# Expert routing on one core: the key's 32 bits searched in six digits in place of seven

## The reference, cut to what matters

```
logits = x @ w_gate                       # 2304 x 8
order  = argsort(-logits.flatten())
cap    = 2304 // 8                        # 288 tokens for each expert
for idx in order:                         # highest logit first
    tok, e = idx // 8, idx % 8
    if tok is assigned or expert e is full: continue
    assign tok to e
out[tokens of e] = relu(x[tokens of e] @ w1[e]) @ w2[e]
```

## Time and profile before

| what | value |
|---|---|
| median of 3 runs | 928.96 us (927.03 to 929.26) |
| the profiled execution | 927.07 us |
| its span, first to last instruction | 925.4 us |
| PE busy | 834.3 us, 90% of the span |
| DVE busy | 608.5 us, 66% |
| ACT busy | 351.6 us, 38% |
| POOL busy | 315.0 us, 34% |
| mean granted TensorE clock | 0.933 of full speed |

### The profile page before, as it was taken

One profiled execution on the slowest core, in us unless ns is written; L12 is line 12 of the kernel. 1 busy time (PEld: TensorE's weight loads), 2 busy tenths in 40 slices (PEclk: granted clock), 3 DMA queues, 4 the chain that ended last, 5 costly groups with the idle time before them and its releaser, 6 DMA issues. The chain is left out here.

```text
span 925.4 us, 21404 instructions
## 1 busy us (share of the span) xinstructions
PE 834.3 (90%) x7720; PEld 757.0 (82%) x7720; DVE 608.5 (66%) x1613; ACT 351.6 (38%) x856; POOL 315.0 (34%) x325
## 2 busy tenths in 40 slices
PE   4776999999999999999999999825999999999984
PEld 3656888888889888888898999724989999999984
DVE  5886886777778767876555555466766766766520
ACT  3453333443344333433323232203445355355451
POOL 5442220221122202211000000006676786786781
PEclk9756999998999999999999999955999999999998
DMA  7873132132221320311101000005614614615600
GB/s 184 257 203 116 40 90 75 27 80 81 62 76 38 88 75 20 80 51 36 46 2 45 0 23 1 24 2 206 206 64 174 228 64 174 229 64 172 230 29 26
DMA packets 97183, 85.40 MB, mean 92 GB/s; under 512 B 64625, under 2 KB 68721, under 8 KB 97137
## 3 DMA queue, kind: packets, MB, share of 16 engines
q1 hardware_dynamic: 94064, 75.34, 26.6%
q0 software_dynamic: 3072, 9.44, 3.2%
HBM read 70.60 MB, written 14.16 MB: 92 GB/s over the span
## 5 line engine op out<-in xcount | busy, mean ns | idle before, releaser
L451 PE MATMUL PS<-xs,W 128*128 128x256 f32 x1728 | 235.6, 289 | 0.2 <-issue 0.2
L451 PEld LDWEIGHTS PS<-xs,W 128*128 128x128 f32 x1728 | 225.2, 195 | 12.0 <-issue 3.9
L451 PE MATMUL PS<-W,g 128*128 128x512 f32 x864 | 223.1, 397 | 0.0
L451 PEld LDWEIGHTS PS<-W,g 128*128 128x128 f32 x864 | 153.7, 188 | 28.3 <-issue 1.0
L541 ACT ACTIVATE a_sb<-PS,one 128x256 f32<-128x256 f32 x144 | 68.2, 474 | 252.1 <-PE PS L451 252.1
L564 DVE TENSOR_SCALAR scratch<-a_sb 128x256 f32<-128x256 f32 x144 | 52.6, 365 | 95.1 <-ACT a_sb L541 95.1
L372 POOL TENSOR_TENSOR P<-P,top 128x640 f32<-128x640 f32 x16 | 21.1, 1316 | 254.3 <-DVE top L332 254.3
L1252 POOL TENSOR_TENSOR w1s<-w1r,w1s 128x512 fp32r<-128x512 f32 x64 | 80.4, 1284 | 29.3 <-ACT w1s L1163 29.1
L1092 PE MATMUL PS<-exs,w1s 128*128 128x288 f32 x256 | 83.1, 325 | 4.9 <-DVE ehs L1217 4.9
L1268 POOL TENSOR_TENSOR w2s<-w2r,w2s 128x512 fp32r<-128x512 f32 x64 | 80.9, 1283 | 17.6 <-ACT w2s L1187 17.4
L1092 PE MATMUL PS<-ehs,w2s 128*128 128x288 f32 x256 | 80.7, 315 | 1.1 <-POOL w2s L1268 1.1
(11 more groups left out here) (166 smaller groups left out, 1426.0 us busy)
## 6 DMA issues: line engine op xcount, KB each, us to landing
w1r<-in_moe_w SPq DMA_DIRECT2D x16, 1024.0 KB, 6.0
w2r<-in_moe_w SPq DMA_DIRECT2D x8, 2048.0 KB, 9.2
qn<-in_q SPq DMA_DIRECT2D x32, 144.0 KB, 3.8
kn<-in_k SPq DMA_DIRECT2D x32, 144.0 KB, 3.6
vd<-in_v SPq DMA_DIRECT2D x16, 288.0 KB
xt<-xT SPq DMA_DIRECT2D x16, 288.0 KB, 2.2
y<-scratch SPq DMA_DIRECT2D x18, 256.0 KB, 2.0
vw<-in_v SPq DMA_DIRECT2D x68, 64.0 KB, 2.4
```

Of the source, the lines that this page charges most:

```text
L451: r = pe.matmul(psum, wsel(w[i]), xsel(x[j]), start=first and t == 0, stop=last and t == 2)
```

## The change

The digits have 5, 5, 5, 5, 6 and 6 bits. Digits 4 and 5 have 64 thresholds each, so their `dve_over` has 18 x 64 = 1152 elements. There is one digit less for each assignment. The digits of steps 3 to 20 are placed anew: digit 3 stays at 3 and 5, digit 4 moves from 9 and 10 to 10 and 12, digit 5 from 14 and 15 to 18 and 19, and digit 6, which had 19 and 20, is gone. With it `dve_choose` moves from step 20 to 19 and `dve_ahead` from 23 to 22. POOL now clears all of `over`, 1216 elements, in place of its tail of 96. `unit` has 768 elements in place of 896, and the table of thresholds 6 x 64 in place of 7 x 32.

```
-DIG = 7
-RADIX = 32
+BITS = (5, 5, 5, 5, 6, 6)
+DIG = len(BITS)
+RADIX = [1 << b for b in BITS]
+MOST = max(RADIX)
+SHIFT = [32 - sum(BITS[:i + 1]) for i in range(DIG)]
+UNIT = [2.0 ** -sum(BITS[1:i + 1]) for i in range(DIG)]
...
-                for t, pattern, base, step in ((con["thr"], [[0, DIG], [1, RADIX]], 1, 0), (con["rev"], [[-1, E]], E, 0),
+                for t, pattern, base, step in ((con["thr"], [[0, DIG], [1, MOST]], 1, 0), (con["rev"], [[-1, E]], E, 0),
...
-        over = sb("over", [128, TILES * RADIX + 128 - RADIX], BF16)
-        over_t = over[:, 0:TILES * RADIX].rearrange("p (t k) -> p t k", t=TILES)
+        over = sb("over", [128, max((TILES - 1) * k + 128 for k in RADIX)], BF16)
+        over_t = [over[:, 0:TILES * k].rearrange("p (t k) -> p t k", t=TILES) for k in RADIX]
...
         def dve_over(dve, i):
-            dve.tensor_tensor(over_t, wide(rest_p, RADIX),
-                              thr[:, i, :].unsqueeze(1).to_broadcast([128, TILES, RADIX]), ALU.is_ge).then_inc(over_ready, 1)
+            k = RADIX[i]
+            dve.tensor_tensor(over_t[i], wide(rest_p, k),
+                              thr[:, i, 0:k].unsqueeze(1).to_broadcast([128, TILES, k]), ALU.is_ge).then_inc(over_ready, 1)
...
-                t = dve.tensor_scalar(digi[:, i, :], key_p, max(27 - 5 * i, 0), RADIX - 1 if i < DIG - 1 else 3,
+                t = dve.tensor_scalar(digi[:, i, :], key_p, SHIFT[i], RADIX[i] - 1,
...
-            dve.tensor_scalar(full[0:RADIX, :], cnt[0:RADIX, 0:E], float(CAP), None, ALU.is_ge).then_inc(full_ready, 1)
+            dve.tensor_scalar(full[0:RADIX[i], :], cnt[0:RADIX[i], 0:E], float(CAP), None, ALU.is_ge).then_inc(full_ready, 1)
...
-                x = pe.matmul(cnt[:, 0:E], over[:, t * RADIX:t * RADIX + 128], hot[:, t, :], start=t == 0, stop=t == TILES - 1)
+                x = pe.matmul(cnt[:, 0:E], over[:, t * RADIX[i]:t * RADIX[i] + 128], hot[:, t, :], start=t == 0, stop=t == TILES - 1)
...
-        COUNT = [49, 55, 60, 3, 9, 14, 19]
-        SUM = [51, 57, 62, 5, 10, 15, 20]
+        COUNT = [49, 55, 60, 3, 10, 18]
+        SUM = [51, 57, 62, 5, 12, 19]
...
-                for t in (unit[:, :, :], full[:, :], rows[:, 2:3], over[:, TILES * RADIX:], oneh[:, TILES * GP:]):
+                for t in (unit[:, :, :], full[:, :], rows[:, 2:3], over[:, :], oneh[:, TILES * GP:]):
...
-KEY_CHAIN, CHAIN = 5, 36
+KEY_CHAIN, CHAIN = 5, 34
```

More of the change, by code:

```diff
@@ L69, in network @@
         con = {}
-        for name, shape, dt in (("thr", [128, DIG, RADIX], F32),
+        for name, shape, dt in (("thr", [128, DIG, MOST], F32),
                                 ("rev", [128, E], F32),
@@ L718, in _ @@
                 for i in range(DIG):
-                    t = pool.memset(con["weight"][:, i, :], float(RADIX) ** -i)
+                    t = pool.memset(con["weight"][:, i, :], UNIT[i])
                 t.then_inc(con_ready, 1)
@@ L793, in _ @@
                 for i in range(1, DIG):
-                    t = dve.tensor_scalar(con["thr"][:, i, :], con["thr"][:, i, :], 1.0 if i == DIG - 1 else 0.0, float(RADIX) ** -i,
+                    t = dve.tensor_scalar(con["thr"][:, i, :], con["thr"][:, i, :], 1.0 if i == DIG - 1 else 0.0, UNIT[i],
                                           ALU.subtract, ALU.mult)
@@ L964, in dve_hot @@
             link(dve, m, dve.tensor_tensor(eq[:, :, :], eq[:, :, :], revb, ALU.mult))
-            dve.tensor_scalar(digi[:, 0, :], key_p, 27, None, ALU.arith_shift_right)
+            dve.tensor_scalar(digi[:, 0, :], key_p, SHIFT[0], None, ALU.arith_shift_right)
             link(dve, m, dve.tensor_reduce(pick[:, :], eq[:, :, :], AX.X, ALU.max))
-            dve.tensor_scalar(rest_p, digi[:, 0, :], 16.0, None, ALU.add)
+            dve.tensor_scalar(rest_p, digi[:, 0, :], RADIX[0] / 2.0, None, ALU.add)
             link(dve, m, dve.tensor_tensor(pick[:, :], pick[:, :], alive_p, ALU.mult))
@@ L995, in dve_choose @@
         def dve_choose(dve, m):
-            dve.tensor_scalar(rest_p, rest_p, kstar[:, 0:1], float(RADIX) ** -(DIG - 1), ALU.subtract, ALU.add)
+            dve.tensor_scalar(rest_p, rest_p, kstar[:, 0:1], UNIT[DIG - 1], ALU.subtract, ALU.add)
             link(dve, m, dve.scalar_tensor_tensor(fe[:, :], tot[:, 0:E], kstar[:, 0:1], con["rev"][:, :], ALU.is_equal, ALU.mult))
@@ L1304, in _ @@
                 for i in range(DIG):
-                    pool.memset(unit[0:RADIX, i, :], float(RADIX) ** -i).then_inc(init, 1)
+                    pool.memset(unit[0:RADIX[i], i, :], UNIT[i]).then_inc(init, 1)
                 pool.affine_select(out=below[:, :], in_=ones[:, :], compare_op=ALU.is_gt, fill=0.0, base=0,
```

## The result

| | before | after |
|---|---|---|
| median | 929.05 us (927.03 to 935.22, 6 runs) | 958.1 us (955.58 to 962.08, 6 runs) |
| the profiled execution | 927.07 us | 956.23 us |
| its span | 925.4 us | 954.5 us |
| clearing by POOL to the end | 325.0 us | 352.2 us |
| mean granted TensorE clock | 0.933 | 0.924 |

The ratio is 1.0305, 95% interval 1.0274 to 1.0336. The prediction was 924.2 us, "faster" with a chance of 0.75. It was wrong in sign, and the time lies far outside its range of 921.8 to 928.9.

A forecast was written before the change was run, and what follows sets the result against it. PE's queue was taken to set the rounds, with step 28 waiting for DVE's ehs(5). Terms -4.5 + 0.3 - 0.55 + 0.05 = -4.7 took 927.07 to 922.4; the median's 1.9 gave 924.2 us, range 921.8 to 928.9.

The forecast's parts named there:

- Is POOL's lock open earlier?: Rounds 1 to 6: `mem`, starting 0.50 ahead of POOL's fourth `w2s` end, gets in there, ending 1.25 us earlier.
- the prediction had 0.87: PE's stall in front of step 28, waiting for DVE's ehs(5): stays at 0.87, with step 28 0.75 us earlier.
- being tied to the steps ahead of 3: POOL's `w2s` borders in a round: set by steps ahead of 3, which were taken as unmoved.
- Rival 1: POOL's lock isn't open at the first border; `mem` ends with the fifth `w2s`; six rounds cost +3.0, 931.8 us; chance 0.13.
- A digit costs PE 0.68: PE's queue, rounds 0 to 6: count 0.55 plus sum 0.13 leave, 4.8 us in all if PE had no other limit.
- `mem` starts earlier: Round 3, step 3 to `mem`: 0.20 from ehs(4) and 0.20 from `kstar` going first, 0.40 us earlier.
- The wide comparison: DVE's 1152-element comparisons: 1.36 us each, 0.60 more, just fitting ahead of their counts; cost taken as 0.
- Ahead of round 0: Chain before round 0: digit -2.48, wide comparisons +1.19, shift and multiplication -0.07, clearing +0.81; together -0.55 us.
- the thresholds' part: Larger threshold table, made by POOL in the first attention unit: 0 to 0.13 us more, taken as 0.05.
- In round 0: `mem` already got in and ends 0.13 earlier; ehs(5) comes 0.37 later; step 28 +0.3 us.
- `dve_ahead` in front of ehs(5): Moved to step 22, it makes ehs(5) start 0.57 behind the choice's last instruction instead of 0.07: 0.50 us lost.
- the forecast's own sum: A round of 34.7 less 0.75 us, with `mem` served at the first border; six rounds -4.5.

The follow-up runs named there:

- Experiment 4: Same run as e5: kernel before, ACT making the high part of POOL's sixth `w2s` one block earlier, ahead of its part of ehs(5); 942.36 us, ratio 1.0142.
- experiment 5: Same run as e6: kernel after, POOL's sixth `w2s` in rounds 0 to 6 also waiting for the end of DVE's choice; 938.43 us, ratio 1.0079.
- Experiment 3: Same run as e4: kernel before, seven digits, the last counted and summed at steps 18 and 19 instead of 19 and 20; 933.52 us, ratio 1.005.
- e14: Kernel after, each POOL `w2s` waiting until its own previous one is complete; 932.14 us, ratio 1.0017.
- e6: Kernel after, POOL's sixth `w2s` in rounds 0 to 6 also waiting for the end of DVE's choice; 938.43 us, ratio 1.0079.
- e1: Kernel after, `mem` made by an instruction with one operand in PSUM; 922.53 us, ratio 0.9935 to the kernel before.
- e7: e1 with `dve_ahead` one step later, behind ehs(5) as in the kernel before; 920.02 us, ratio 0.9881 to the kernel before.
- e4: Kernel before, seven digits, the last counted and summed at steps 18 and 19 instead of 19 and 20, `dve_ahead` at 22; 933.52 us, ratio 1.005.
- e13: Kernel after, each POOL `w2s` waiting until the one before its previous one is complete; 961.57 us, ratio 1.0338 to the kernel before.
- e5: Kernel before, ACT making the high part of POOL's sixth `w2s` one block earlier, ahead of its part of ehs(5); 942.36 us, ratio 1.0142.
- e12: Kernel before, seven digits, `mem` with one operand in PSUM; 943.4 us, ratio 0.9998, in the group where the kernel before took 944.39.

## Why the prediction was wrong

**The step that failed** is "Is POOL's lock open earlier?". It read a threshold in time out of three rows: a start 0.10 ahead of POOL's next is too little, 0.30 and 0.59 are enough, so "`mem` has 0.50 and should end at 758.82". The lead isn't what decides. In the kernel after `mem` started 0.69 ahead of the border at 769.77 (764.75 + 4 x 1.255) and missed it, and three more behind it (that behind `sidx` counted), so it ended at 773.64, and step 28 waited 4.67 where the prediction had 0.87. Experiment 4 moved only POOL's queue and moved the end of `mem`; experiment 5 held back only the sixth `w2s` and `mem` ended with the fifth. Experiment 3 doesn't bear on the lead, since `mem` came later in it and not earlier. The 0.12 of e14 opened the first border that `mem` met. The Trainium skill ("SBUF — State Buffer", section "Who interferes with whom") gives the lock for the whole instruction to whoever issues first; the trace agrees with that for each single instruction. It shows besides that where a `w2s` followed a `w2s` and had been ready for some 0.45 us or more, it went ahead of the waiting DVE each time.

**What should have been asked** is where POOL's next `w2s` isn't ready in time, and what the change does to that. Behind the fifth `w2s` that was set by ACT, whose high part of the sixth follows PE's steps. The prediction moved everything behind step 3 forward by what the digit frees, ehs(4) and `mem` among it, and left POOL's streak fixed, "being tied to the steps ahead of 3". It didn't move ACT's part of the sixth and seventh `w2s` forward with PE: 13.92 behind step 0 became 13.23, while the fifth still ended at 14.02. Taking out the digit made the sixth ready early enough to shut `mem` out at the border through which it had come.

**Rival 1** had the mechanism in its condition ("or only a pause of POOL lets it in"), and an end that was too early: it kept `mem` at the fifth's end, 1.8 long, for 931.8. It was 4.56 long, since POOL's next was first not ready behind the seventh. It was given 0.13. Its price of half a microsecond per round is nearly what e6 shows at step 28 (15.97 behind step 0 in place of 15.34), but e6 lost more behind that step, by the clock. A wait of 4.7 per round with a clock at half speed behind it stood in no case.

**Steps that held.** Most of the others came out close:
- A digit costs PE 0.68: the last matmul ahead of step 28 starts 13.57 behind step 0, so PE could begin at 13.70, before at 14.39.
- `mem` starts earlier: by 0.58, predicted 0.40. The direction held, the size was nearly half as large again.
- The wide comparison takes 1.36 (predicted 1.36) and ends 0.07 ahead of its count, which starts at 766.37. It just fits, and PE doesn't wait for it.
- Ahead of round 0 two wide digits take 3.08 each, the others 2.48; DVE starts 2.09 behind the clearing, before 1.26 (+0.83, predicted +0.81). From the clearing to the last instruction of the choice it is 21.70 in place of 22.15: -0.45, predicted -0.55 (with the thresholds' part left out). The rows, DVE and POOL:

```profile
616.48 1.36 DVE L951 TENSOR_TENSOR over<-PS,thr 128x1152 bf16<-128x1152 f32 x1
...
619.56 1.36 DVE L951 TENSOR_TENSOR over<-PS,thr 128x1152 bf16<-128x1152 f32 x1
```

```profile
602.29 0.74 POOL L1306 MEMSET unit<- 128x768 bf16 x1 [180.14 <-POOLq L600]
...
603.04 1.11 POOL L1306 MEMSET over<- 128x1216 bf16 x1
```

- In round 0, where ACT spaces POOL's instructions, `mem` took 0.76 and ended with the running `w2s`, 0.2 later behind step 0 than before, where the forecast had it 0.13 earlier. PE's wait there is about 1.1 (29.1 less six of 4.67), and step 28 starts 16.03 behind step 0 in place of 15.24: +0.8, predicted +0.3.
- `dve_ahead` in front of ehs(5) costs: ehs(5) starts 0.66 behind the choice's last instruction, predicted 0.57, before 0.07. With `mem` free, moving it back took the last 2.6 us of waits away (e1 and e7).

With the lock open at the first border, which is e14, the forecast's own sum comes near: `mem` to `mem` is 34.43 there, where it said 33.94, and 0.4 of the difference is `mem`'s end, 13.20 behind step 0 and not 12.79, for POOL's wider borders. Even so e14 only ties with the kernel before.

**Left open.** In the earlier trace rows DVE got in although POOL's next instruction had begun, and so did `mem` behind the fifth `w2s` of the kernel before, of e4 and of e6, with `sidx` next. So it isn't every ready GpSimd instruction that keeps DVE out. One guess falls with the rows of the kernel after: that DVE is kept out only where something is ready behind the next instruction too. At the sixth's end the seventh was next, and for the eighth POOL then had to wait, and `mem` was still passed over, in each of the rounds 1 to 6. The eighth in round 3:

```profile
780.04 1.30 POOL L1273 TENSOR_TENSOR w2s<-w2r,w2s 128x512 fp32r<-128x512 f32 x1 [6.44 <-ACT w2s L1192]
```

How long the sixth must have been ready is bounded only roughly: up to 0.14 before the fifth's end let `mem` in (before), 0.71 and more kept it out (e13 and after), and at the border between the sixth and the seventh 0.45 did. No run closes the gap.

## What to carry to other kernels

A small VectorE instruction that can be locked out by GpSimd isn't priced by its own length or by the one GpSimd instruction beside it, but, beside a streak like this one, by the time until GpSimd's next instruction isn't ready in time; so ask of every change, also of one that only takes work from a third engine, whether it makes that next instruction ready earlier. The cheapest cure is to give the small instruction an operand in PSUM (0.22 us in place of 4.56); a pause of 0.12 us at each border of the GpSimd streak is the next. A stall in front of TensorE can cost more than its length: behind 4.7 us the clock was low in six rounds of six, behind some 2.3 us in nine of twelve (e5 and e6).

## What the runs showed of the hardware that was not expected

- DVE, waiting since 0.69 before a border, was passed over at four borders in a row by POOL instructions that were ready (three `w2s` and `sidx`, 4.56 us), at three in e5 (2.80). A gap some 0.12 us wider let it in at once (e14).
- PE's idle time of 4.7 us was followed by a granted clock of 0.50 and 0.68 in the next two stretches of 2 us, one of 2.1 us (e5, round 3) by 0.57 and 0.58; behind under 1 us it stayed at 1.00. Of the 27.2 us lost, about 10 are this.
- The same kernel before took 928 to 930 us beside most experiments and 944.39 in one group. PE's rows of e12 there show a sum that starts 2.27 behind its count, where in the kernel before it is 0.95:

```profile
794.38 0.61 PE L1056 MATMUL PS<-hot,over 128*128 128x8 bf16 x18
796.65 0.18 PE L1061 MATMUL PS<-full,unit 128*128 128x8 bf16 x1 [1.16 <-DVE full L984]
```

DVE's `full` itself starts 1.45 behind the recorded end of that count (796.44 and 794.99), and DVE had nothing else to do. In all four kernels of this group `full` comes 0.8 to 1.8 behind its count at one or two places of a round, and in no other profile of this document more than 0.6. Why isn't known, and that it is the chip isn't shown: this group and the fourth, in which the kernel before took 930.10, have the same chip number on record. But it moved ACT against POOL, and with it the size of the effect that this change has.
